# One-tile block of an attention and MoE kernel: row copies to VectorE, last waits to SyncE, first block count given sooner

## The reference

```python
y[:, :, t] = scale * einsum(q[:, :, t], state)          # attention with decay, rows x of 512
e_idx = argmax(x @ w_gate + modality_bias[modality_id]) # one expert for each row
out[mask] = gate_w[mask, None] * (maximum(x[mask] @ w1[e], 0) @ w2[e])   # 512 -> 1024 -> 512
h = (x @ w1) * (x @ w2) @ w3 ; return h @ w_out         # moe2, 512 -> 1024 -> 1024 -> 512
```

## Time and profile before

| | us |
|---|---|
| median of 3 runs (856.77 to 857.12) | 856.78 |
| the profiled execution: its own time | 857.94 |
| its span in the trace | 855.9 |
| PE busy | 823.2 (96%) |
| DVE busy | 420.0 (49%) |
| ACT busy | 288.9 (34%) |
| POOL busy | 173.3 (20%) |

### The profile page before, as it was taken

How to read it: one execution, slowest core, us unless ns; L and a number is a source line. 1 busy time by engine, 2 the same in 40 slices (tenths; PEclk the granted TensorE clock), 3 DMA queues, 4 the chain that set the end, 5 groups by cost and what they waited for, 6 DMA issues and landing times.

```text
span 855.9 us, 14864 instructions
## 1 busy us (share of the span) xinstructions
PE 823.2 (96%) x5578; PEld 703.1 (82%) x5579; DVE 420.0 (49%) x662; ACT 288.9 (34%) x467; POOL 173.3 (20%) x207
## 2 busy tenths in 40 slices
PE   9999999998999999999997799999999999999995
PEld 8899888787999998888885588788888788888784
DVE  3578698621212234121235778752587732687400
ACT  2234423421322333212235544423444423444210
POOL 2222002202022020202011333211334122432011
PEclk9999999999999999999998899999999999999998
DMA  9999891323031152202132111241121321111010
GB/s 344 336 333 300 288 354 50 148 100 101 1 99 49 49 196 98 92 6 50 49 123 75 37 51 50 68 137 43 60 64 50 115 83 49 50 50 49 13 50 37
DMA packets 51456, 91.88 MB, mean 107 GB/s; under 512 B 8529, under 2 KB 15313, under 8 KB 51409
## 3 DMA queue, kind: packets, MB, share of 16 engines
q1 hardware_dynamic: 41728, 68.47, 23.5%
q0 software_dynamic: 4736, 14.72, 5.2%
q10 hardware_dynamic: 4946, 8.08, 2.7%
HBM read 71.03 MB, written 20.22 MB: 107 GB/s over the span
## 4 chain that ended last, share of the span: by engine, by line
PE 89%; DVE 4%; issue 3%; ACT 2%; ACTq 1%; DMA 0%; DVEq 0%; POOL 0%; SPq 0%
PE bank L444 34%; PE attn L444 34%; PE pair L444 7%; PE bank L969 3%; PE attn L996 3%; PE pair L981 3%; PE pair L1074 2%; PE bank L1008 1%; PE attn L987 1%; PE bank L946 1%; PE bank L1157 1%; ACTq L393 1%; DVE w3T L1253 0%; DMA w_raw<-in_moe_w_dram 0%; ACT yhi L667 0%
## 5 line engine op out<-in xcount | busy, mean ns | idle before, releaser
L444 PE MATMUL bank<-xT,we_p 128*128 128x512 f32 (+1 forms) x672 | 140.7, 370 | 3.9 <-issue 2.6
L444 PE MATMUL attn<-hT,we_p 128*128 128x512 f32 (+1 forms) x672 | 141.8, 368 | 0.0
L444 PEld LDWEIGHTS bank<-xT,we_p 128*128 128x128 f32 x672 | 123.3, 190 | 20.9 <-issue 5.0
L444 PEld LDWEIGHTS attn<-hT,we_p 128*128 128x128 f32 x672 | 121.3, 188 | 14.4
L444 PE MATMUL attn<-wc,gT 128*128 128x512 f32 x576 | 131.1, 389 | 0.0
L444 PEld LDWEIGHTS attn<-wc,gT 128*128 128x128 f32 x576 | 108.1, 188 | 22.5
L1499 DVE SCALAR_TENSOR_TENSOR hT<-bank,hT 128x512 fp32r<-128x512 f32 x56 | 38.7, 691 | 150.6 <-ACT hT L741 150.6
L444 PE MATMUL bank<-yhi,whi 128*128 128x512 f32 x240 | 95.6, 398 | 7.0 <-issue 3.4
L444 PE MATMUL bank<-yhi,wlo 128*128 128x512 f32 x240 | 94.6, 394 | 0.0
L667 ACT ACTIVATE whi<-w_raw 128x768 fp32r<-128x768 f32 (+1 forms) x72 | 50.3, 700 | 62.6 <-DMA w_raw<-in_moe_w_dram 33.0
L741 ACT ACTIVATE hT<-bank 128x512 fp32r<-128x512 f32 x56 | 33.5, 599 | 102.2 <-PE bank L444 102.2
(11 more groups left out here) (198 smaller groups left out, 1209.7 us busy)
## 6 DMA issues: line engine op xcount, KB each, us to landing
we_raw<-in_moe_w_dram SPq DMA_DIRECT2D x6, 2048.0 KB, 9.0
w_raw<-in_moe_w_dram SPq DMA_DIRECT2D x40, 256.0 KB, 2.7
yT_sorted<-yout ACTq DMA_DIRECT2D x7, 1024.0 KB, 4.6
qkv<-in_q_t_dram SPq DMA_DIRECT2D x24, 256.0 KB, 3.5
qkv<-in_v_dram SPq DMA_DIRECT2D x24, 256.0 KB, 5.2
x_rows<-x_keep SPq DMA_DIRECT2D x24, 256.0 KB, 3.6
qkv<-in_k_t_dram SPq DMA_DIRECT2D x23, 256.0 KB, 5.1
qkv<-in_k_dram SPq DMA_DIRECT2D x20, 256.0 KB, 5.5
```

The lines of the kernel that those rows point to most:

```text
L444: i = pe.matmul(out_, left(a), right(b), start=(first and n == 0), stop=(last and n == 2), **kw)
```

## The change

In the one-tile block the two copies to `h_rows` go from ACT to DVE. They are signalled on `s_hlo` and no longer on `s_hhi`, and the counts are shared out anew so that each half still gives four on both semaphores. DVE does copy 0 ahead of all LO pieces of w2, then piece 0, copy 1, the LO relu of half 0, piece 1, the LO relu of half 1, pieces 2 and 3. ACT does pieces 0 and 1, both relus, pieces 2 and 3. Each engine has one branch for a window with a new expert and one for the other case, where it had two small branches around the pieces.

`dve.sem_inc(s_hlo, 2)` stands ahead of `wc_lo(6)`. PE's wait for `s_wclo` ahead of its loop is gone. The waits for the last scatters stand at the end of SP's stream and not of POOL's.

```diff
@@ block.sync, at its end
+            for i in range(2):
+                sp.wait_ge(s_out[i], 16 * NT // 2)
@@ block.gpsimd, at its end
-            for i in range(2):
-                pool.wait_ge(s_out[i], 16 * NT // 2)
@@ block.scalar
                 def one_tile_hidden():
-                    this = is_new(act, w)
-                    if_new(act, this, w, lambda run: w2_hi(run, range(0, 2)))
-                    for half in range(2):
-                        act.wait_ge(s_hp, w * KF + (half + 1))
-                        copy(h_rows[:, half * BANK:(half + 1) * BANK], bank[half][:, :]).then_inc(s_hhi, 1)
-                    for half in range(2):
+                    def relu(half):
                         act.wait_ge(s_hp, w * KF + (half + 1) * (GT - 1) + 2)
                         act.activation(hT[:, HI, half * GT:(half + 1) * GT, 0:P], bank[half][:, :].rearrange("p (f t) -> p f t", f=GT),
-                                       ACT.Relu).then_inc(s_hhi, GT - 1)
-                    if_new(act, this, w, lambda run: w2_hi(run, range(2, 4)))
+                                       ACT.Relu).then_inc(s_hhi, GT)
+
+                    this = is_new(act, w)
+                    with act.If(this > 0):
+                        run = table(act, w, RUN_OF, 0, E - 1)
+                        w2_hi(run, range(0, 2))
+                        relu(0)
+                        relu(1)
+                        w2_hi(run, range(2, 4))
+                    with act.If(this < 1):
+                        relu(0)
+                        relu(1)
@@ block.tensor
                     for half in range(2):
-                        pe.wait_ge(s_hhi, w * KF + (half + 1))
+                        pe.wait_ge(s_hlo, w * KF + (half + 3))
                         for t in range(GT):
                             i = pe.transpose(bank[half][:, t * P:(t + 1) * P], h_rows[:, half * BANK + t * P:half * BANK + (t + 1) * P], ident)
                         i.then_inc(s_hp, GT - 1)
                     pe.wait_ge(s_y, w * KD + 1)
                     for f in range(KF):
                         if f % GT == 0:
-                            pe.wait_ge(s_hlo, w * KF + (f + GT + 2))
+                            pe.wait_ge(s_hlo, w * KF + (GT + (f // GT + 1) * (GT - 1)))
...
             pe.wait_ge(s_tab, 1)
-            pe.wait_ge(s_wclo, KF - 2)
             each_window(pe, window)
@@ block.vector
             w1_lo(0, early_chunks(5))
+            dve.sem_inc(s_hlo, 2)
             wc_lo(6)
...
                 def one_tile_hidden():
-                    this = is_new(dve, w)
-                    if_new(dve, this, w, lambda run: w2_lo(run, range(0, 2)))
-                    for half in range(2):
-                        dve.wait_ge(s_hhi, w * KF + (half + 1) * (GT - 1) + 2)
+                    def rows_copy(half):
+                        dve.wait_ge(s_hp, w * KF + (half + 1))
+                        dve.tensor_copy(h_rows[:, half * BANK:(half + 1) * BANK], bank[half][:, :]).then_inc(s_hlo, 1)
+
+                    def relu_lo(half):
+                        dve.wait_ge(s_hhi, w * KF + (half + 1) * GT)
                         fs = slice(half * GT, (half + 1) * GT)
                         dve.scalar_tensor_tensor(hT[:, LO, fs, 0:P], bank[half][:, :].rearrange("p (f t) -> p f t", f=GT), 0.0,
-                                                 hT[:, HI, fs, 0:P].bitcast(F32), ALU.max, ALU.subtract).then_inc(s_hlo, GT)
-                    if_new(dve, this, w, lambda run: w2_lo(run, range(2, 4)))
+                                                 hT[:, HI, fs, 0:P].bitcast(F32), ALU.max, ALU.subtract).then_inc(s_hlo, GT - 1)
+
+                    this = is_new(dve, w)
+                    with dve.If(this > 0):
+                        run = table(dve, w, RUN_OF, 0, E - 1)
+                        rows_copy(0)
+                        w2_lo(run, (0,))
+                        rows_copy(1)
+                        relu_lo(0)
+                        w2_lo(run, (1,))
+                        relu_lo(1)
+                        w2_lo(run, (2, 3))
+                    with dve.If(this < 1):
+                        rows_copy(0)
+                        rows_copy(1)
+                        relu_lo(0)
+                        relu_lo(1)
...
-            dve.sem_inc(s_hlo, 2)
             each_window(dve, window)
```

## The result

| | before | changed |
|---|---|---|
| median, us (lowest to highest, 4 executions each) | 856.88 (856.77 to 857.12) | 851.62 (850.51 to 853.90) |
| ratio, 95% interval | | 0.9941 (0.9912 to 0.9969) |
| profiled execution: own time / span | 857.94 / 855.9 | 853.90 / 852.2 |

The kernel became 5.3 us faster. 7.6 us had been forecast (849.2 us); 851.6 lies inside the stated range, near its middle, and 2.4 us above the forecast.

What follows compares the result with a forecast made beforehand. PE was taken as the bound (89% of the span), so only its idle or half-clock time counts. 5.8 us for counts, copies and clock plus 1.8 for the last waits made 7.6: 856.78 to 849.2 us, range 848.0 to 853.5.

Steps and rivals of the forecast that it cites:

- Counts, 0.93: Window 0: counts given sooner remove PE's whole wait ahead of its first product, 0.93 us (bounds 0 and 0.93).
- Copies, 1.1 us earlier (0.9 to 1.3): Window 7, the one-tile block: with the copies on DVE, the w2 product starts 1.1 us sooner.
- The clock in the product: w2 product in window 7: its length depends on half clock following PE's shortened idle gap of about 2.1 us.
- The three outcomes: w2 product: no clock fall, 5.6 us; one half-clock stretch, 7.2 us; both stretches as before, 8.5 us.
- What that reaches: Product's end to a_sum and quad(1): a_sum sooner by 3.85, 2.5 or 1.1 us; sums 5.5, 4.15 or 1.1.
- The floor that DVE's own work sets: Window 7: DVE's own nearly unbroken work keeps a_sum from coming before 479.55 in the old frame.
- The term behind quad(1), 1.65 us: Behind quad(1): a shorter gap keeps the clock up, 10 matmuls in 3.3 us become 14.5, gaining 1.65 us.
- The last waits, 1.8: Kernel end: POOL's 5.31 us DRAIN starts sooner with the waits on SP; 1.8 us gained (bounds 0 and 1.85).
- Rival 1: Kernel end: DRAIN counted from the scatters' landing, so no gain there, the rest as forecast; 851.0 us, chance 0.20.
- Rivals 2 and 3: Window 7: clock falls as before, 853.0 us, chance 0.15; with DRAIN counted from landing too, 854.8 us, chance 0.10.
- rival 4: Window 7: copy 1 behind LO piece 0 brings no more than ACT's order; only 0.93 left, 855.9 us, chance 0.05.
- Rival 5: Window 7: new code layout stalls ACT's or DVE's sequencer on the path to copy 1; up to 859.8 us, chance 0.04.

Runs made afterwards that it cites:

- f1_gap: Changed kernel plus 8 idle matmuls on PE between the transposes of half 0 and half 1: median 850.0 us, ratio 0.9926.
- r_order: Changed kernel with DVE's copy 1 ahead of its first LO piece and ACT's relu of half 0 between its pieces 0 and 1: median 848.69 us, ratio 0.9893.
- e3_tail: Kernel before with only the last scatter waits moved from POOL to SP: median 856.07 us, ratio 0.9982.
- e1_counts: Kernel before with only the s_hlo counts given ahead of wc_lo(6) and PE's s_wclo wait removed: median 854.74 us, ratio 0.9979.
- e2_copies: Kernel before with only the changed kernel's one-tile block on ACT, DVE and PE: median 855.01 us, ratio 0.9966.
- f2_loop: Changed kernel plus 4 idle 32-bit matmuls on PE behind the transposes of y_rows: median 850.48 us, ratio 0.9909.
- r_again: The r_order kernel run once more, next to the changed kernel on one chip: median 850.14 us, ratio 0.9887 against the kernel before.
- rf_both: The r_order kernel plus the four idle 32-bit matmuls of f2_loop: median 848.50 us, ratio 0.9874.
- a_again: The changed kernel run again, unaltered, beside its three parts made alone: median 851.89 us, ratio 0.9940 against the kernel before.

## Why the prediction came out as it did, step by step

**Counts, 0.93.** Right: no gap at window 0 in any profile with the edit, and the rows' LO parts held nothing up. That PE then starts window 0 at 157.64 and not 0.9 sooner is no loss of this gain. The work before window 0 ended between 155.4 and 157.8 us in the various kernels, though none of them had altered it.

**Copies, 1.1 us earlier (0.9 to 1.3).** Right: 1.20 (10.01 to 8.81). The copy took 0.69 where 0.65 was assumed, and the four transposes ran right behind the hidden layer. Half of the 1.15 us of the eight in the earlier trace rows is 0.58 and not 0.65; 0.60 was measured. The remaining idle time of 2.17 us was forecast as 2.1.

**The clock in the product.** The three outcomes were drawn rightly, and the second came, in every profile of the changed kernel and of the copies alone: 7.2 to 7.35 us. The gap of 2.17 costs one stretch, as the earlier trace rows's 2.35 did. The choice failed here: the forecast put 0.7 us on the chance that it costs none, halfway between "none" and "one". By its nearest row there was no ground for that half. The later profiles show how little one row says here: of the four gaps of 2.31 to 2.39 us behind window 0, only the one of the earlier trace rows was followed by a stretch.

**What that reaches.** Right for that outcome: `a_sum` 2.5 us sooner was worked out, 2.4 to 2.5 measured. The floor that DVE's own work sets, 479.55 in the old frame, is real too: in f1_gap `a_sum` follows that work without idle time, at 479.8 in the same frame.

The gap ahead of `quad(1)` was forecast at about 1.3 and measured at 1.35, 1.50 and 1.51, and the clock stays up behind it, as the row of the 1.47 gap had said. The number owes something to luck. PE's last factors of `quad(0)` were to be held by DVE's LO parts until 482.3 (old frame). They did end there (at 483.83 in the changed trace, which is 1.5 us behind the old frame at window 7), but by the LO parts alone they would have ended sooner. In r_order PE waits for the LO part `wlo`, and its 13th matmul of `quad(0)` starts 0.15 us behind that part's end:

```profile
470.54 0.94 DVE L1257 TENSOR_TENSOR wlo<-w_raw,whi 128x768 fp32r<-128x768 f32 x1
```

```profile
471.63 0.47 PE L444 MATMUL bank<-yhi,whi 128*128 128x512 f32 x1 [0.46 <-DVE wlo L1257]
```

In the changed trace the same part ends at 477.39 (first line), and the 13th matmul starts at 478.18 (second line), 0.64 us later than it could:

```profile
476.45 0.94 DVE L1256 TENSOR_TENSOR wlo<-w_raw,whi 128x768 fp32r<-128x768 f32 x1
```

```profile
478.18 0.41 PE L444 MATMUL bank<-yhi,whi 128*128 128x512 f32 x1
```

What holds it is the second stretch of 3.4 us at half clock, and no outcome of the forecast had that stretch. Without it the gap ahead of `quad(1)` would have been about 2.0 us (an estimate, 1.35 + 0.64), between the 1.67 behind which the clock stayed up and the 2.76 behind which it fell.

Half-clock time of each profile, us, by the granted clock:

| | hidden layer to product's end | from there to quad(1) | behind quad(1) |
|---|---|---|---|
| old block: before, e3_tail | 6.8 | 3.4 | 3.4 |
| old block: e1_counts | 6.8 | 6.8 | 0 |
| new block: changed (three profiles), e2_copies, fewer scatters | 3.4 | 6.8 | 0 |
| f1_gap | 0 | 10.2 | 0 |
| f2_loop | 3.4 | 3.4 | 0 |
| r_order | 0 | 3.4 | 0 |
| r_again | 0 | 6.8 | 0 |
| rf_both | 0 | 0 | 0 |

So the new block has 3.4 us less of it than the old one, and not the 6.8 that the forecast's second outcome counted. Even with the old block the stretch behind `quad(1)` can be missing, as in e1_counts.

**The term behind quad(1), 1.65 us.** This is the term that was mis-sized. The stretch of half clock behind `quad(1)` is gone, and PE's matmuls there do run 1.5 to 1.6 us sooner behind the start of `quad(1)`. But they were counted to the end of the kernel as if nothing else had been waiting on their way. PE meets a wait that it was too late for before; in a_again, 14.29 us behind the start of `quad(1)`:

```profile
483.63 0.50 PE L444 MATMUL bank<-yhi,whi 128*128 128x512 f32 x1 [1.51 <-DVE wlo L1256]
...
497.92 0.50 PE L444 MATMUL bank<-yhi,whi 128*128 128x512 f32 x1 [0.39 <-ACT p_one L666]
```

From the first `a_sum` to the second it was 7.39 us before, and 6.02, 6.57 and 6.58 in the three profiles of the changed kernel: 0.8 to 1.4 gained, not 1.65. (e1_counts, with the old block but no stretch behind `quad(1)`, has 6.58 too.) From the first to the last of the 24 it was 309.80, against 309.03, 309.46 and 309.69: 0.1 to 0.8 left, 0.4 in the mean. (e3_tail, with the stretch, has 309.61, and e2_copies, without it, 308.61, so 0.4 is within what executions differ by.) That the rest is used up in small waits of the later steps is the likely reading; which of them took how much was not separated. Beside it stands the time of the copies alone, 2.6 us with an error of 0.5, of which 2.49 are there by the first `a_sum`. The forecast's own count for this term, 10 matmuls that become 14.5, would give only 1.0 us at 0.23 us a matmul; its 1.65 is half of the 3.3 us.

**The last waits, 1.8.** Right: 1.95 to 2.0 by the tails, 1.55 with an error of 0.6 by the clock of the whole. Rival 1, which counted the DRAIN from the landing, is out, by the tail and by the kernel with fewer scatters. The Trainium skill ("VectorE: DVE Perf Modes", section "The DRAIN you can't avoid") gives some 12 ns for such a DRAIN on every engine. In the changed kernel SP's took 7 ns, but ACT's 717, DVE's 730 and PE's 4267, and POOL's took 5306 to 6507 ns over all profiles. Following the page would have cost this term.

**The sum.** 0.93 + 2.4 + 0.4 + 1.95 = 5.7 from the stretches that can be told apart, beside 5.3, 5.7 and 6.2 measured as differences of medians. The forecast's 7.6 had 0.7 too much from the choice of clock and 1.25 too much from the term behind `quad(1)`; the two make up the difference. Rivals 2 and 3 needed an unchanged clock and rival 4 a window 7 that gains nothing, and neither is in a trace. Rival 5's code stall isn't either: DVE's copy 0 waits 12.08 us for PE and not for its own sequencer, and copy 1 follows the LO piece at once.

**The width.** The range's own arithmetic gave the forecast case 848.5 to 849.9. That was too narrow, since it allowed no error for a term counted from row to end of kernel, nor for the median of a kernel whose executions spread by several us; the wide range held only thanks to the rivals.

## What to carry to other kernels

A gap that PE stands in costs itself and can cost half clock behind it, so ask for each gap that is shortened whether it is still long enough for that; shorten it further or fill it with matmuls into a free bank if it is. Then look where the half-clock time went: it can come back a few microseconds later, which is a gain only if PE has idle time there. A stretch gained in the middle of a pipeline is worth its full length only until the next wait that used to be hidden: follow it there before it is carried to the end. Give the last waits of a kernel to an engine that does nothing else, and let the engine with the long DRAIN be done first.

## What the runs showed of the chip that was not expected

- POOL's closing DRAIN ended 4.6 to 5.5 us after POOL's last instruction or wait, whether that was a scatter or a sum, in every profile here. It lasted 5306 ns behind a wait, 6507 ns behind an issue and 5944 ns behind a sum, and in the last two cases it began at most 0.3 us before that instruction's start.
- The clock fell for about 3.4 us, 6.8 us or, once, 10.2 us at a time. Gaps of 2.76 and 2.83 us ahead of `quad(1)` were followed by it, gaps of 1.33 to 1.67 weren't (seven profiles). Behind window 0, gaps of 2.31 to 3.76 us had no stretch, one or two, and the longer gap not always the more. Ahead of the seventh matmul of `quad(0)` a gap of 1.80 us (f2_loop) was followed by one, a gap of 1.72 (rf_both) wasn't: the length of one gap alone doesn't decide.
- The same kernel's executions differ by more than its first four showed (856.77 to 857.12). The kernel before lay between 852.4 and 863.0 in 35 later executions. Against that spread one profile beside another decides nothing outside the stretches that the edit touches.
- PE's idle time between windows 0 and 1 was 2.31 to 3.76 us in thirteen profiles, and the branch of its sequencer there took 3.3 to 4.2 us, though nothing near it was altered.
